# Channel-mix start with one eight-product unit instead of two, statistics ahead of the mix, and another order of GpSimd's sums

## The reference, cut to what matters

```
q_pool = q.reshape(B, H, S // 2, 2, D).mean(axis=3)          # B 4, H 8, S 1152, D 64
attn = softmax(q_pool @ k^T / sqrt(D));  x = attn @ v        # x: (4, 576, 512)
xn = (x - mean) / sqrt(var + 1e-6) * g_ln                    # per token, over 512 channels
out = x + relu(xn @ w_ch1) @ w_ch2                           # 512 -> 2048 -> 512
```

## Time and profile before

| what | us |
|---|---|
| median of 3 runs (lowest, highest) | 813.0 (812.87, 813.71) |
| the profiled execution's own time | 812.01 |
| its span, first to last instruction | 810.3 |
| PE busy | 796.0 |
| DVE busy | 643.2 |
| ACT busy | 417.7 |
| POOL busy | 446.1 |

### The profile page before, as it was taken

One profiled execution on the slowest core, in us unless ns is written; L12 is line 12 of the kernel. 1 busy time (PEld: TensorE's weight loads), 2 busy tenths in 40 slices (PEclk: granted clock), 3 DMA queues, 4 the chain that ended last, 5 costly groups with the idle time before them and its releaser, 6 DMA issues. The chain is left out here.

```text
span 810.3 us, 17080 instructions
## 1 busy us (share of the span) xinstructions
PE 796.0 (98%) x6488; PEld 665.4 (82%) x6488; DVE 643.2 (79%) x990; ACT 417.7 (52%) x941; POOL 446.1 (55%) x341
## 2 busy tenths in 40 slices
PE   8999999999999999999999999999999999999998
PEld 6777778787778777788779899989888989999897
DVE  6788888888898999888567967898877788766654
ACT  4676556675566765667723445453335444432431
POOL 3988898888898888887794212331321333122100
PEclk9999999999999999999999999999999999999999
DMA  8566443566444665311112121213321122421212
GB/s 187 133 146 142 118 90 95 140 146 145 100 95 99 146 146 129 76 62 51 32 53 63 62 86 53 63 56 105 116 66 53 53 92 66 142 79 56 62 40 78
DMA packets 39681, 75.36 MB, mean 93 GB/s; under 512 B 8880, under 2 KB 23472, under 8 KB 36016
## 3 DMA queue, kind: packets, MB, share of 16 engines
q1 hardware_dynamic: 38128, 73.88, 34.9%
q10 hardware_dynamic: 1472, 0.39, 0.3%
HBM read 69.54 MB, written 4.72 MB: 92 GB/s over the span
## 5 line engine op out<-in xcount | busy, mean ns | idle before, releaser
L579 POOL TENSOR_TENSOR acc<-acc,pT 128x576 f32<-128x576 f32 x160 | 238.4, 1490 | 23.2 <-ACT pT L911 0.4
L1261 PE MATMUL banks<-w2f,hT 128*128 128x512 f32 x864 | 214.3, 393 | 0.0
L911 ACT ACTIVATE pT<-banks 128x576 f32<-128x576 f32 x288 | 171.8, 653 | 36.8 <-PE banks L711 31.2
L1261 PEld LDWEIGHTS banks<-w2f,hT 128*128 128x128 f32 x864 | 160.3, 188 | 28.8 <-issue 0.2
L1021 DVE TENSOR_REDUCE pm<-banks 128x2 f32<-128x1024 f32 x128 | 153.2, 1221 | 37.3 <-PE banks L657 36.0
L713 PE MATMUL banks<-qT,kT 64*128 64x288 f32 x1728 | 162.1, 298 | 3.4 <-DVE pm L1021 2.3
L713 PEld LDWEIGHTS banks<-qT,kT 64*128 64x128 f32 x1728 | 133.5, 184 | 18.7 <-DVE pm L1021 7.5
L724 PE MATMUL banks<-pT,vn 128*64 128x288 f32 x1152 | 146.1, 408 | 0.0
L1339 ACT ACTIVATE hT<-mid 128x384 fp32r<-128x384 f32 x88 | 46.4, 527 | 184.1 <-DVE mid L1406 182.8
L391 POOL TENSOR_TENSOR w_sums<-w_stage 128x256 f32<-128x256 f32 x22 | 17.2, 783 | 211.1 <-DMA w_stage<-in_moe_w_ch_dram 211.1
L1406 DVE TENSOR_TENSOR mid<-banks,mid 128x384 f32<-128x384 f32 x154 | 85.5, 555 | 57.4 <-PE banks L1250 53.4
(11 more groups left out here) (120 smaller groups left out, 973.2 us busy)
## 6 DMA issues: line engine op xcount, KB each, us to landing
q_in_rows<-in_q_dram SPq DMA_DIRECT2D x56, 284.0 KB, 6.5
k_in_rows<-in_k_dram SPq DMA_DIRECT2D x56, 284.0 KB, 5.1
w_stage<-in_moe_w_ch_dram SPq DMA_DIRECT2D x24, 512.0 KB, 3.8
w_stage<-in_moe_w_ch_dram SPq DMA_DIRECT2D x48, 256.0 KB, 2.7
vn<-in_v_dram SPq DMA_DIRECT2D x16, 576.0 KB, 5.0
out_dram<-x SPq DMA_DIRECT2D x16, 256.0 KB, 3.2
q_in_rows<-in_q_dram SPq DMA_DIRECT2D x4, 256.0 KB, 3.1
k_in_rows<-in_k_dram SPq DMA_DIRECT2D x2, 288.0 KB, 4.1
```

The source lines that it names most:

```text
L579: nc.gpsimd.tensor_tensor(total, pT[:, h % 2, 0] if kt == 1 else total, pT[:, h % 2, kt], ALU.add).then_inc(chained, 1)
L911: nc.scalar.activation(pT[:, h % 2, kt], pair_banks("S", n)[:, :, 0:HW], ACT.Exp, scale=SCALE).then_inc(exp_done, 1)
L1261: last = nc.tensor.matmul(banks[:, k % 2 * (CT // 2) + kk], hT[:, k, a, tokens], w2f[:, (2 * u + k // 2) % 4, b], start=p == 0 and k < 2 a ...
```

## The change

It sets PLAIN from 2 to 1, so that unit 1 is worked with seven products. The statistics of part 1 (six tiles, their moments and the variance) move on DVE from units 1 and 2 to a place ahead of the mix, behind the last but one `scale_outputs`; those of part 2 stay. POOL makes the sums of weights of unit 1 first, then T1 to T4, then the sums of weights of unit 2. The high and low parts of T1 and T2 stand at the end of unit 0, those of T3 and T4 inside unit 1: T3's low part behind the addition 11, T4's behind the addition 22.

```diff
-    PLAIN = 2
+    PLAIN = 1
...
             scale_outputs(j - 1)
+            dve.wait_ge(x_written, 3 * PAIRS // 4)
+            for kk in range(CT):
+                statistics(1, kk)
+            moments_of(1)
+            variance_eps(1)
...
         def mix_gpsimd(pool):
-            sum_tokens(nc.gpsimd, pool, 0, T1)
-            sum_tokens(nc.gpsimd, pool, 0, T2)
             pool.wait_ge(scored, KT * HALVES)
             sum_weights(nc.gpsimd, pool, PLAIN)
-            sum_tokens(nc.gpsimd, pool, 0, T3)
-            sum_tokens(nc.gpsimd, pool, 0, T4)
-            for u in range(1, UNITS):
+            for i in (T1, T2, T3, T4):
+                sum_tokens(nc.gpsimd, pool, 0, i)
+            sum_weights(nc.gpsimd, pool, PLAIN + 1)
+            for u in range(PLAIN, UNITS):
...
                 second_hi(2 * u + 1)
-                for i in ((T2, T1), (T3,))[u]:
+                for i in (T1, T2):
                     tokens_hi(act, nc.scalar.copy, 0, i)
...
                 first_copy(u)
-                if u == PLAIN:
-                    tokens_hi(act, nc.scalar.copy, 0, T4)
                 next_hi(u, 0, 1)
                 if turns:
                     scale_tokens(*turns[0], banks[:, 7])
+                if u == PLAIN:
+                    tokens_hi(act, nc.scalar.copy, 0, T3)
                 hidden_hi(u, 0)
+                if u == PLAIN:
+                    tokens_hi(act, nc.scalar.copy, 0, T4)
                 next_hi(u, 1, 2)
...
-                if p == 1:
+                if p == 1 and n > 1:
                     dve.wait_ge(x_written, PAIRS)
...
-                if p == 2:
+                if p == 2 and n > 1:
                     statistics(n, 4)
...
                 second_lo(2 * u + 1)
-                for i in ((T2, T1), (T3,))[u]:
+                for i in (T1, T2):
                     tokens_lo(nc.vector, dve, 0, i)
-                next_tokens(u)
             for u in range(PLAIN, UNITS):
                 middle(u, "V")
                 next_lo(u, 0, 1)
                 middle(u, "11")
                 if u == PLAIN:
-                    tokens_lo(nc.vector, dve, 0, T4)
+                    tokens_lo(nc.vector, dve, 0, T3)
...
                 middle(u, "22")
+                if u == PLAIN:
+                    tokens_lo(nc.vector, dve, 0, T4)
                 next_lo(u, 3, 4)
```

## The result

| | before | changed |
|---|---|---|
| median of 7 runs, us (lowest, highest) | 813.0 (812.41, 813.71) | 815.31 (814.83, 816.36) |
| profiled execution's own time | 812.01 | 814.83 |
| its span | 810.3 | 813.1 |
| mean granted clock over the span | 1.000 | 0.997 |

The changed kernel is 2.3 us slower: ratio 1.0033, 95% interval 1.0024 to 1.0043. The forecast was 815.9, slower.

What follows compares the result with a forecast made beforehand. PE, busy 796.0 of 810.3 us, was taken as the bound. Delays of 6.2 us (3.5 + 0 + 1.0 + 1.7) less 3.02 gave +3.2, taken as +2.9: 815.9 against the median, range 812.4 to 817.8.

Steps and rivals of the forecast that it cites:

- The work taken off: Units 1 and 2 on PE: seven products save 1.23 us, moved statistics 1.79 us of stall, together at most 3.02.
- The cover of the statistics: DVE ahead of the mix: 4.4 us of statistics from 414.44 fit idle time of 6.44, 2.0 to spare, costing nothing.
- The gate: Unit 1: down(0, 0) waits for DVE's scaled outputs, due at 429.5, starts at 432.5; PE idles 2.5 to 3 us.
- Product 1: Unit 1: waits for T2's low part, starts at 435.0 where due was 431.5; delay so far 3.5 us.
- Products 5 and 6: Unit 1: product 5 waits for V5, 1.0 us late; product 6 for T4's low part, 1.7 more.
- the rival in which the gain lands: Scaled outputs come by 429.5, no first delay, only 0.85 us left for T4's low part: 810.9 us; chance 0.1.
- the first delay: Unit 1 up to product 1, behind the late down(0, 0): 3.5 us, bounds 2.0 and 4.0.
- The total: Whole kernel: delays 6.2 less 3.02 give +3.2 us, bounds -0.2 and +4.3; +2.9 taken.

Runs made afterwards that it cites:

- e1: The kernel before with only the statistics of part 1 moved ahead of the mix, two plain units and the old POOL order kept; 810.95 us against 812.53, ratio 0.9979.
- e2: The changed kernel with the statistics put back into units 1 and 2; ratio 1.0029 to the kernel before.
- e6: The changed kernel with POOL's sums T1 and T2 made earlier, in a gap of the attention part; 817.6 us, ratio 1.0056 to the kernel before.
- e5: The changed kernel with 20 identity transposes keeping PE busy between product 0 of unit 1 and down 0; ratio 1.0033 to the kernel before.
- e3: The changed kernel with the last take_end, scale_outputs and second_lo(0) ahead of the low parts of S3, S4 and A22 on DVE; 815.85 us, ratio 1.0048 to before.
- e8: e7 with DVE's work in unit 0 reordered, low parts of T1 and T2 ahead of those of S1, S3, S4; 814.16 us against 812.23 for the kernel before.
- e10: e5 with T1's low part ahead of the last take_end and scale_outputs on DVE; 813.78 us, ratio 1.0011 to the kernel before.
- e4: The changed kernel with POOL's old order, T1 and T2 ahead of unit 1's sums of weights; 817.26 us against 812.23 for the kernel before.
- e9: The changed kernel with T1's low part ahead of the last take_end and scale_outputs on DVE; 815.26 us, ratio 1.0029 to the kernel before.
- e7: The changed kernel with POOL's sums of weights for unit 2 moved ahead of T3; 815.94 us, ratio 1.0045 to the kernel before.

## Why the prediction was right, and where it was not

- **The work taken off.** Forecast 3.02 us: 1.23 for the product form, 1.79 for unit 2's stall. Both went: unit 2 takes 15.59 us (449.94 to 465.53). But the reason given for the 1.79 was only part of the cause. Moving the statistics is enough by itself (e1) and not needed in the changed kernel (e2), where V and all behind it come sooner after the unit's start. So in the changed kernel the 1.79 would have gone without the step that the prediction gives as their cause.
- **The cover of the statistics.** As forecast, with less room: 414.48 to 419.48, 1.4 us to spare instead of 2.0.
- **The gate.** Step by step as forecast, within 0.15 us: S1's low part ends at 428.3 (428.4), product 0 starts at 428.91 (429.0), L836 ends at 432.26 (432.4), down 0 starts at 432.41 (432.5). The wait ahead of down 0 is 2.2 us, a little under the 2.5 to 3 that were given as a sign. e6 confirms that the meeting with POOL's sums makes the gate late.
- **Product 1.** The term was mis-sized: 4.4 us late instead of 3.5. I held T2's low part for the last to come (434.9; it came at 434.73) and left out that a wait of 2.2 us can halve the clock; down 0 took 3.48 instead of 2.06. The slow clock also took 0.2 us more on the next twelve matmuls. e5 removes exactly this.
- **Products 5 and 6.** Forecast 1.0 and 1.7 late behind product 1; measured 0 and 1.2, so of the waits given as signs ahead of products 1, 5 and 6 only the last is there. V5 came at 444.01 (444.2 forecast) and product 6 at 446.74 (447.15). Since the chain runs from T1's low part and not from product 1, what product 1 lost more the later waits lost less. That is why the sum, a delay of 5.9 (449.94 less 444.06, the unit of 15.68 from 428.38) against 6.2, came out nearly right, though one term was too small and others too large. It isn't luck: the prediction placed V5 and T4's low part by the times of DVE and POOL, so what it missed at product 1 dropped out of its sum again. But its bounds and the rival in which the gain lands treat the first delay and the later ones as if each could be won by itself, and that rival calls the gate "the one mechanism"; e5 and e3 show that the gate's share alone is worth nothing.
- **The total.** +2.8 in the profile against +2.9 forecast, +2.3 in the medians. The rows gave +3.2; what came in below that is DVE's work up to T4's low part, which ended at 446.64 instead of 447.0. The 0.3 taken off in the forecast was a guess of that. The rival in which the gain lands needed `down(0, 0)` by 429.5, and L836 ended at 432.26. e3 shows that a gate 1.4 us sooner, with T1's low part where it was, wins nothing, which that rival had left out.
- **What stays open.** Whether one plain unit can be faster than two. The nearest here, e8 and e10, are still 1.1 and 1.4 us behind the kernel before in the stretch, and 2.9 and 3.2 behind e1. An own place for T3 and T4, which would cut the chain at its head, wasn't tried.

The version to keep is e1: the statistics ahead of the mix, everything else as before, 0.21% faster (0.12 to 0.29).

## What to carry to other kernels

Take the parts of a change apart before believing their sum: here one part wins 1.7 us by itself and the other loses 2.3, and a stall with two causes is won only once. Fewer matmuls help only where the engines that feed them have slack; six matmuls saved (1.05 us) brought three more low parts, four sums on POOL and a later gate. When a removed wait gives nothing, look for a second chain that arrives at the same time, measured from a point that the edit did not move (12.54 us in three kernels).

## What the runs showed of the hardware

- The granted clock fell to half, from 2.4 to 1.2 GHz, after single waits of PE of 2.2 us (changed kernel, e2), 2.65 (e4), 3.1 (e9) and 3.4 (e7). In the changed kernel and e9 the first matmuls behind the wait were still fast (1.00 from 433.47 to 434.50 in e9), in e4 and e7 the clock was 0.50 from the first. Nine matmuls of 512 columns took 3.48 us instead of 2.06 (changed kernel), twelve of 384 took 3.73 instead of 2.10 (e4).
- It did not fall after waits of 0.8 and 1.6 us (e3), 1.3 (e4 and e6, ahead of down 0) or 1.0 and 1.4 (e8). A wait of 0.6 us and one of 1.3 behind it, ahead of products 5 and 6, halved it in e6 but not in e3, e4 and e5, where the same two waits stand. So for waits of this size the length of a wait alone did not decide. e6 shows a fall in the attention part too, where the mean clock from 416.0 to 421.5 was 0.80 behind waits of 0.8 and 1.0 us.
- `variance_eps`, a DVE instruction with one small SBUF input, took 0.90 us at 418.58 instead of 0.17 while POOL added. It ended at 419.48, where POOL's addition ended (419.46). The six bn_stats beside the same additions took 3.66 us, as fast as alone (four took 2.47 at 448.50 of the kernel before, with POOL idle). The Trainium skill (SBUF — State Buffer, "Who interferes with whom") states that tensor_scalar can take the shared port pair in a two-port mode; the trace agrees, with those 0.90 us, which the prediction had at 0.17.
